# Attention and two expert layers on one core: chunks of 256 instead of 384 tokens, another order of the attention, and K, V and weights brought in differently

## What is computed

```
B, H, S, D = 2, 8, 768, 64; block, window = 32, 16
k_sum = max of k over blocks of 32;  v_sum = mean of v over blocks of 32       # 24 of each
scores = [q k^T / 8 inside |i-j| < 16, else -1e9 ;  q k_sum^T / 8 + log(32)]
x = softmax(scores) @ [v ; v_sum]            -> 1536 tokens x 512
h = relu(x @ w_in)      (512 -> 2048);  y = (h * h) @ w_out        (2048 -> 512)
h2 = y @ w2_in          (512 -> 1024);  solu = h2 * softmax(h2)
out = layernorm(solu) * g @ w2_out           (1024 -> 512)
```

## Time and profile before

| | before |
|---|---|
| median of 3 runs | 531.06 us |
| span of the profiled execution | 529.4 us |
| TensorE busy (share of span) | 492.2 us (93%) |
| VectorE, ScalarE, GpSimd busy | 268.0, 223.8, 36.2 us |
| first layer pair (the chunks' matmuls) begins to run without a gap | about 62.7 us |
| third layer begins | 378.7 us |

### The profile page before, as it was taken

How to read it: one execution, slowest core, us unless ns; L and a number is a source line. 1 busy time by engine, 2 the same in 40 slices (tenths; PEclk the granted TensorE clock), 3 DMA queues, 4 the chain that set the end, 5 groups by cost and what they waited for, 6 DMA issues and landing times.

```text
span 529.4 us, 8722 instructions
## 1 busy us (share of the span) xinstructions
PE 492.2 (93%) x3088; PEld 436.5 (82%) x3088; DVE 268.0 (51%) x548; ACT 223.8 (42%) x553; POOL 36.2 (7%) x45
## 2 busy tenths in 40 slices
PE   3346699999999999999999999999999999999997
PEld 2235499999989999989999999999987888888875
DVE  5456276576575455564644454355374444444330
ACT  3345366556464444453443443333243233333331
POOL 0005411211100000000000000000010000000000
PEclk9966599999999999999999999999999999999999
DMA  7367453342450311232210034222062112211011
GB/s 228 114 207 273 140 156 87 120 140 79 138 181 36 95 36 64 87 133 93 79 40 1 1 104 165 69 61 59 21 195 64 60 62 79 78 60 59 22 39 40
DMA packets 29783, 49.82 MB, mean 94 GB/s; under 512 B 2272, under 2 KB 16864, under 8 KB 29248
## 3 DMA queue, kind: packets, MB, share of 16 engines
q1 hardware_dynamic: 23424, 30.65, 18.9%
q10 hardware_dynamic: 4608, 8.39, 5.4%
q0 software_dynamic: 1728, 10.49, 5.3%
HBM read 40.08 MB, written 9.44 MB: 94 GB/s over the span
## 4 chain that ended last, share of the span: by engine, by line
PE 91%; issue 4%; DVE 2%; DMA 1%; ACT 0%; SPq 0%; ACTq 0%
PE bank L790 27%; PE bank L765 26%; PE bank L896 13%; PE bank L917 13%; PE bank L726 5%; PE bank L746 3%; PE bank L735 2%; PE bank L908 2%; DMA v_raw<-vT 1%; DMA q_sb<-qT 0%; DVE k_ext L535 0%; PE bank L754 0%; DVE k_sum L540 0%; DVE neg_max L557 0%; DVE probs L553 0%
## 5 line engine op out<-in xcount | busy, mean ns | idle before, releaser
L790 PE MATMUL bank<-h_hi,wout_hi 128*128 128x384 f32 x256 | 91.1, 356 | 0.4 <-DVE h_lo L610 0.4
L765 PE MATMUL bank<-x_hi,win_hi 128*128 (+1 forms) x256 | 90.2, 352 | 0.8 <-DVE x_lo L574 0.8
L765 PE MATMUL bank<-x_hi,win_lo 128*128 (+1 forms) x256 | 86.9, 339 | 0.0
L765 PE MATMUL bank<-x_lo,win_hi 128*128 (+1 forms) x256 | 86.8, 339 | 0.0
L790 PE MATMUL bank<-h_hi,wout_lo 128*128 128x384 f32 x256 | 86.4, 337 | 0.0
L790 PE MATMUL bank<-h_lo,wout_hi 128*128 128x384 f32 x256 | 86.1, 336 | 0.0
L409 ACT ACTIVATE relu<-bank 128x384 f32<-128x384 f32 x64 | 31.4, 490 | 103.4 <-PE bank L765 101.4
L607 DVE TENSOR_TENSOR relu<-relu 128x384 f32<-128x384 f32 x64 | 35.7, 558 | 64.9 <-ACT h_hi L414 64.9
L355 ACT ACTIVATE probs<-probs,neg_max 128x118 f32<-128x118 f32 x96 | 36.8, 384 | 42.7 <-DVE neg_max L557 42.7
L790 PEld LDWEIGHTS bank<-h_hi,wout_hi 128*128 128x128 f32 x256 | 48.0, 188 | 5.1 <-issue 3.9
L726 PE MATMUL bank<-k_ext,q_sb 64*64 64x118 f32 x384 | 31.4, 304 | 21.8 <-issue 16.1
(11 more groups left out here) (66 smaller groups left out, 776.7 us busy)
## 6 DMA issues: line engine op xcount, KB each, us to landing
wstage<-wtiles ACTq DMA_DIRECT2D x32, 256.0 KB, 2.7
k_raw<-kT SPq DMA_DIRECT2D x16, 399.0 KB, 3.1
v_raw<-vT SPq DMA_DIRECT2D x16, 384.0 KB, 3.4
v_ext<-vwin SPq DMA_DIRECT2D x16, 282.0 KB
w_in_raw<-w_in_c POOLq DMA_DIRECT2D x4, 1024.0 KB, 6.8
q_sb<-qT SPq DMA_DIRECT2D x16, 192.0 KB, 9.3
y_dram<-x_hi POOLq DMA_DIRECT2D x4, 768.0 KB, 3.8
y_dram<-x_lo POOLq DMA_DIRECT2D x4, 768.0 KB, 4.7
```

The lines of the kernel that those rows point to most:

```text
L765: last = nc.tensor.matmul(bank[:, 6 + f % 2, 0:CH], win[a][:, f * WC + k * P:f * WC + (k + 1) * P], rhs, start=(k == 0 and a == 0 and b == ...
L790: last = nc.tensor.matmul(bank[:, 2 + d, 0:CH], wout[a][:, f * WC + d * P:f * WC + (d + 1) * P], h[b][:, f % 2, :], start=(f == 0 and a == ...
```

## The change

What it does:

- CH is 256 instead of 384, so there are 6 chunks of 16 slices, and every `up` and `down` is 12 matmuls of 256 columns. A unit of attention is one pair of heads and one chunk (TPU = 4 tiles; 24 units).
- Four units come first, then the scores of a fifth. The other attention work stands in `SLOTS`: at slice-steps 0, 4, 7, 10, 13 and from 16 on at each fourth, values of unit a, scores of unit c and transposes of unit b, one behind the other.
- `up(n + 2)` is issued in step n ahead of `down(n)`; `h_hi` and `h_lo` have three slots, the squares of VectorE a buffer `sqr` of their own.
- K is loaded once a batch and pair; windows and summaries of K are spread by GpSimd. V's block sums come from a table `vblk` in which 96 partitions hold the blocks of four pairs; the means are spread into `v_ext` by transfers from `v_mean`; TensorE's turning of the sums and ScalarE's spreading fall away.
- All weights of the first layer pair are loaded whole from SyncE's queue in groups of two tiles (512 KB), into the memory of their own low parts, and the low part is written over the raw one (GpSimd for `w_in`, VectorE for `w_out`, ScalarE the high parts). The third layer's weights come the same way, a group after each two `up` of the last chunk.
- Tiles 8 to 11 of the third layer read y where it was made; only the first four chunks go through DRAM.
- All loops are written out; every engine runs straight code.

The core of the diff (the functions of VectorE and ScalarE for a unit keep their operations, on 4 tiles in place of 3; a line "..." marks what is left out):

```diff
-CH = 384
+CH = 256
-TPJ = CH // QT
-TPU = 3
+TPU = CH // QT
+UNITS = PPB * NCHUNK
+SLOTS = {0: (None, 4, 5), 4: (4, 5, 6), 7: (5, 6, 7), 10: (6, 7, 8), 13: (7, 8, 9)}
+for _u in range(8, UNITS):
+    SLOTS[4 * (_u - 4)] = (_u, _u + 1 if _u + 1 < UNITS else None, _u + 2 if _u + 2 < UNITS else None)
...
 # SyncE's queue
+            load_k(0, 0)
+            load_q(0)
+            sp.dma_start(mask[:, :], mask_c).then_inc(mask_in, 16)
+            load_k(0, 1)
+            sp.dma_start(ident[:, :], ident_c).then_inc(ident_in, 16)
+            load_vf(0)
+            load_q(1)
+            load_vf(1)
+            load_k(0, 2)
+            load_q(2)
+            load_vw(0)
+            load_k(0, 3)
+            load_q(3)
+            load_vw(1)
+            load_w(win_raw, w_in_t, 0, win_in)
+            load_vw(2)
+            load_vw(3)
+            sp.wait_ge(vmean_ok, 1)
+            for p in range(PPB):
+                spread_v(p)
+            sp.wait_ge(scores_ok, 1)
+            load_q(4)
+            load_w(wout_raw, w_out_t, 0, wout_in)
+            load_w(win_raw, w_in_t, 1, win_in)
...
 # ScalarE
+            def hidden(n):
+                act.wait_ge(up_ok, n + 1)
+                if n >= 2:
+                    act.wait_ge(sq_ok, n - 1)
+                nc.scalar.activation(relu[:, n % 2, :], up_bank(n), ACT.Relu).then_inc(relu_ok, 1)
...
+            def x_high(u):
+                c, p = u // PPB, u % PPB
+                act.wait_ge(attn_ps, u + 1)
+                if c >= 2:
+                    act.wait_ge(y_saved[c % 2], 32 * (c // 2))
...
 # TensorE
+            def values(u):
+                c, p = u // PPB, u % PPB
+                pe.wait_ge(vw_in[p], 16 * (c + 1))
+                pe.wait_ge(vs_in[p], 16 * (u // UPB + 1))
+                pe.wait_ge(probsT_ok, u + 1)
+                if u >= 1:
+                    pe.wait_ge(xlo_ok, u)
...
+            scores(0)
+            scores(1)
+            turned(0)
+            scores(2)
+            turned(1)
+            values(0)
+            scores(3)
+            turned(2)
+            values(1)
+            turned(3)
+            values(2)
+            scores(4)
+            up(0, range(0, 2))
+            values(3)
+            up(0, range(2, 3))
+            up(1, range(0, 3))
+            up(0, range(3, 4))
+            up(1, range(3, 4))
+            for n in range(STEPS - 2):
+                if n in SLOTS:
+                    a, b, c = SLOTS[n]
+                    if a is not None:
+                        values(a)
+                    if c is not None:
+                        scores(c)
+                    if b is not None:
+                        turned(b)
+                up(n + 2)
+                down(n)
```

More of the change, by code:

```diff
@@ L159, in build, with scores_bank, up_bank, down_bank @@
         o_ps, o_ok = sem("o_ps"), sem("o_ok")
[L160 to L209, removed]
+        def scores_bank(u):
+            return bank[:, 0 if u % 2 == 0 else 3, 0:UC]
+        probsT_bank = bank[0:KX, 1, 0:TPU * P]
+        xT_bank = bank[:, 2, 0:CH]
+        def up_bank(n):
+            return bank[:, 6 + n % 2, 0:CH]
+        def down_bank(d):
+            return bank[:, 4 + d // 2, (d % 2) * CH:(d % 2 + 1) * CH]
+        def h2_bank(i):
+            return bank[:, 2 * (i % 2):2 * (i % 2) + 2, :].rearrange("p b c -> p (b c)")
+        lnT_bank = bank[:, 6:8, :].rearrange("p b c -> p (b c)")
+        def tile_cols(f):
+            return slice(f * WC, (f + 1) * WC)
         block = ctx.enter_context(nc.Block())
@@ L248, in _ @@
[L248 to L259, removed]
@@ new lines, in store @@
+            def store(i):
+                sp.wait_ge(o_ok, i + 1)
+                sp.dma_start(out[i * P:(i + 1) * P, :], o_sb[:, i % 2, :]).then_inc(o_out[i % 2], 16)
+            sp.wait_ge(xlo_ok, UNITS)
+            for c in range(2):
+                sp.wait_ge(y_saved[c], 32)
+            load_y(0)
+            load_y(1)
+            for g in range(F1 // WG):
+                load_w2(g)
+            for c in range(2):
+                sp.wait_ge(y_saved[c], 64)
+            for i in range(TT):
+                if 2 <= i + 2 < (NCHUNK - 2) * TPC:
+                    sp.wait_ge(h2_ok, i + 1)
+                    load_y(i + 2)
+                store(i)
@@ new lines, in _ @@
+            windows_k(4)
+            w_in_low(0)
+            w_in_low(1)
+            windows_k(5)
+            w_in_low(2)
+            w_in_low(3)
+            for n in range(LAST):
+                if n % F1 == 0 and n:
+                    save_y(n // F1 - 1)
+                if n + 4 < F1:
+                    w_in_low(n + 4)
+                if n in SLOTS and SLOTS[n][2] is not None and SLOTS[n][2] + 1 < UNITS:
+                    u = SLOTS[n][2] + 1
+                    if UPB <= u < UPB + PPB:
+                        summaries_k(1, u - UPB)
+                    windows_k(u)
@@ new lines, in _ @@
+            w_in_high(1)
+            x_high(2)
+            x_high(3)
+            exps(4)
+            w_in_high(2)
+            w_out_high(0)
+            hidden(0)
+            w_in_high(3)
+            w_out_high(1)
+            hidden(1)
+            for n in range(STEPS):
+                if n % F1 == 0 and n:
+                    chunk_y(n // F1 - 1)
+                if n in SLOTS:
+                    a, b, c = SLOTS[n]
+                    if b is not None:
+                        copy_probsT(b)
+                    if a is not None:
+                        x_high(a)
+                if n - 1 in SLOTS and SLOTS[n - 1][2] is not None:
+                    exps(SLOTS[n - 1][2])
+                if n + 2 < STEPS:
+                    hidden(n + 2)
+                if n + 2 < F1:
+                    w_out_high(n + 2)
+                if n + 4 < F1:
+                    w_in_high(n + 4)
+                if n >= LAST + 2:
+                    w2_high(n - LAST - 2)
@@ new lines, in _, with scores @@
+            win, wout, x, h = (win_hi, win_lo), (wout_hi, wout_lo), (x_hi, x_lo), (h_hi, h_lo)
+            def scores(u):
+                c, p = u // PPB, u % PPB
+                pe.wait_ge(q_in[p], 16 * (c + 1))
+                pe.wait_ge(kwin_ok, u + 1)
+                pe.wait_ge(kbc_ok, (u // UPB) * PPB + p + 1)
+                if u >= 2:
+                    pe.wait_ge(masked_ok, u - 1)
+                out_ = scores_bank(u)
+                for t in range(TPU):
+                    for e in range(2):
+                        rows = slice(e * D, (e + 1) * D)
+                        last = nc.tensor.matmul(out_[e * QT:(e + 1) * QT, t * KX:(t + 1) * KX],
+                                                q_sb[rows, p, t * QT:(t + 1) * QT],
+                                                k_ext[rows, p, t * KX:(t + 1) * KX],
@@ new lines, in down @@
+            def down(n):
+                c, f = n // F1, n % F1
+                if c == 0:
+                    pe.wait_ge(wout_lo_ok, f + 1)
+                pe.wait_ge(hlo_ok, n + 1)
+                for d in range(KD):
+                    if f == 0 and c and d % 2 == 0:
+                        pe.wait_ge(yclo_ok, 2 * c - 1 + d // 2)
+                    for a, b in PASSES:
+                        last = nc.tensor.matmul(down_bank(d), wout[a][:, f * WC + d * P:f * WC + (d + 1) * P],
+                                                h[b][:, n % 3, :],
+                                                start=(f == 0 and a == 0 and b == 0 and d % 2 == 0),
+                                                stop=(f == F1 - 1 and a == 1), skip_group_check=True)
+                last.then_inc(down_ok, 1)
```

992 lines of the change are left out of this document (436 added, 556 removed).

## The result

The changed kernel takes 582.11 us (median of 4 runs, 579.98 to 583.03) where the kernel before takes 531.17 (4 runs, 530.66 to 532.26): ratio 1.094, 95% interval 1.092 to 1.096. It is 51 us slower; the forecast was 517, the range 504 to 531. The profiled execution has a span of 578.2 us.

The account below looks back on a forecast made before the run. Until the start ends latencies and transfers decide, then the distance between matmuls. Start 53 + matmuls 268.4 + attention 43.1 + chunk waits 2 + third layer 148.6 = 515.1, plus 1.7 from profiled run to median: 517 us, range 504 to 531.

Parts of the forecast that it names:

- Third layer: The last stage: same matmuls and transposes a tile, nothing waiting for squares or weights, so 148.6 us as before.
- Hand-overs: Chunk starts, where the first x_high waits for y's transfers: just holds, 2 us in all, bounds 0 and 8.
- rival 3: Waits of 3 us a chunk boundary and 3 in the first chunk, or 0.122 a matmul: 524 to 528, chance 0.2.
- signs named as wrong: Pieces of 12 matmuls above 1.49; TensorE idle for ReLU or low parts every sixteenth step; start over before 45 or after 60.
- Start: Before the step loop: transfers decide, values(0) waits until 35.5 us, then 17.5 more, so the loop starts at 53.
- Matmuls: Step loop: 2280 matmuls of 256 columns at 0.1177 us each, 268.4 us; 262 at 0.115, 278 at 0.122.
- The line through two sizes: Price of a 256-column matmul drawn from the measured 384 and 512 columns: 0.1177 us, the value taken.
- the upper bound: Price of a 256-column matmul keeping the 384-column excess of 0.0155 as a fixed cost: 0.122 us.
- The load as the floor: A weight load takes 0.11 us beneath one matmul, so it can be the floor, under 0.1177 by 7%.
- Attention: Beside the step loop's matmuls: 20 units at 2.2 us, less 0.9 for missing scores, 43.1 us; bounds 39 and 54.
- Up two steps ahead: Step loop: two steps, 5.6 us, cover the chain behind an up, so the old 2.4 us gap before the last chunk's first down goes.
- ScalarE in the first chunk: ScalarE needs 2.9 us a step where TensorE needs 3.5, so its work is covered, by 0.6 only.

Follow-up runs that it names:

- x1_yload: The changed kernel with SyncE's third-layer queue storing tile i - 2, not tile i, before it loads y of tile i + 3: 540.56 us.
- b2_store: b1_pad with the changed kernel's third-layer SyncE order (load of tile i + 2, store of tile i, load of tile i + 3): 588.35 us.
- x7_ypad: x1_yload with the V rows of the windows padded from 94 to 96 partitions, attention left at its own steps: 521.5 us.
- x3_both: The changed kernel with the later store of x1_yload and attention at steps 4, 7, 10, 13 of a chunk instead of 0, 4, 8, 12: 529.52 us.
- c1_narrow: x3_both with matmuls of 192 columns in up and 240 in down from the second chunk on, part of the result not computed: 515.53 us.
- c2_apart: x3_both with a slot's attention apart: scores ahead of up, transposes between up and down, values behind down: 546.81 us.
- x6_sums: x5_start with VectorE's sums of K for the second batch one step earlier: 512.4 us.
- b1_pad: The kernel before the change with the V rows of the windows padded from 94 to 96 partitions, nothing else: 512.69 us.
- x5_start: x4_pad with the start reordered so that scores and transposes of later units run ahead of the first values: 514.65 us.
- x4_pad: x3_both with the V rows of the windows padded on the host from 94 to 96 partitions: 520.92 us.

## Why the prediction was wrong, and where it held

**Third layer: the step that failed.** "Same 48 matmuls and 8 transposes a tile ... 148.6 again." It walked TensorE's work, the weights' split and VectorE's maximum, and not SyncE's queue, though the diff rewrites the loop that fills it. Two lines of code and the earlier trace rows would have been enough: a tile takes some 12 us (two products of 5.60 and the transposes), `store(i)` can go out only when tile i is done, `load_y(i + 3)` is behind it, issue and landing are some 5 us, and tile i + 3 is due at once, because TensorE runs ahead. None of the rivals had it. `x1_yload` takes the loss away, `b2_store` makes it: shown from both sides. It is 38.8 of the 63 us missed.

**Hand-overs: mechanism right, size wrong.** The order ScalarE, ReLU, TensorE, its place (each sixteenth step) and the thin margin stood in the text; rival 3 gave it 3 us a boundary. ScalarE was to be free 7 us after the last `down` and was so after 11.3. Landing was taken as 4 us, from the 4.7 of the earlier trace rows for more bytes; it was 8.1 to 9.0. The text had the two slow engines for the start and did not ask what else is on them when y goes out: a `vwin` load issued in the same step. `x7_ypad` shows it, and so does `x3_both`, where no `vwin` load is issued beside y and its low part lands in 3.7, 4.1 and 5.1 us at the same three hand-overs: about the 4 us that had been reckoned. And a TensorE that stands still for 4 us gets the clock back late, a cost that the sum held only for the start: 6.2 of the 16.9 us. The point is one of the signs named as wrong, idle time put down to ReLU at every sixteenth step, here at three of the four.

**Start: right to 0.6 us, with a wait behind it that the sum did not have.** `values(0)` was put at 35.5 and ran at 36.78, with the DMA engines at a tenth and 33 to 66 GB/s from 22 to 27 us; padding moved it by 8. The rest was to take 17.5 and took 16.8. But `turned(4)`, in the loop's first slot, then waited for VectorE's normalisation, which stood behind the low part of the first `w_out` (1.34), and at 58.6 the clock fell for 3.3 us. The prediction's walk of the first chunk looked at ScalarE alone; its rival 3 had 3 us there.

```profile
53.56 1.03 PE L699 MATMUL bank<-k_ext,q_sb 64*64 64x118 f32 x16
57.38 0.66 PE L712 MATMUL bank<-ident,probs 128*118 128x128 f32 x4 [2.79 <-DVE probs L547]
```

**Matmuls: right within its bounds.** 12 in 1.44 us and not 1.41, 0.120 where the text had 0.115, 0.1177 and 0.122. The line through two sizes undershot by 0.0023; the upper bound, a fixed cost on top of the columns, was 0.002 too high. 5.2 us over 2280. The load as the floor at 0.110 was right, and 0.010 below. The Trainium skill, TensorE: Matmul & The Clock Gate, Part 3, The mechanism, says in one line that loads overlap matmuls only where the row groups differ, and in another that a load into the background weight buffer is pulled ahead too. `c1_narrow` contradicts the first again, with 0.110 a pair where load plus stream would be 0.19; the second would fit.

**Attention: right.** 2.15 a full unit against 2.2, and `c2_apart` gives the 0.24 that a unit saves by standing in one place. The chain of the changed kernel, one unit:

```profile
71.03 0.62 PE bank L725 x16
71.64 0.96 PE bank L699 x16
72.60 0.58 PE bank L712 x4
```

**Up two steps ahead, ScalarE in the first chunk: right.** No `down` waits for ReLU or squares, and behind its first slot the first chunk's steps have no gap.

**What the change is worth without its faults.** Its own structure costs 2304 x 0.120 = 276.5 us of matmul where 1536 x 0.1755 = 269.6 stood, and gives back attention and the gap of 2.4. `x6_sums`, all faults removed, is 512.4; `b1_pad`, the kernel before with two partitions of zeros, is 512.7. Both are some 3.5% under the kernel before, and no difference between them is shown. The largest gain of all runs was in one transfer's shape, open to the old kernel as well. That the two run equally fast through different stages is measured; that a start like that of `x5_start` in the kernel before would put it ahead is not tried.

## What to carry to other kernels

Walk every queue in program order, not only the engine that bounds the kernel: a load issued behind a store that waits for compute is as late as that compute. Before anything else, look in the DMA view for stretches at a tenth or two of the engines, and make the partition count of such a transfer a multiple of 16; ask also which other transfers share its engines. Price a stillstand of TensorE with the slow matmuls that follow it.

## What the runs showed of the hardware

- A load on two engines delays others that use all sixteen: y's landing went from 9.04 to 5.52 us when a `vwin` load of 188 KB beside it was padded by 4 KB. The issuing queue is held up too: behind the first two `vwin` loads of the start one issue of SyncE took 5.43 us and the next two 5.75 (below); in `x4_pad` the same took 0.43 and 3.00.

```profile
11.10 5.43 SPq L208 DMA_DIRECT2D win_raw<-w_in_t  x1
16.57 5.75 SPq L194 DMA_DIRECT2D v_ext<-vwin  x2
```

- After stillstands of 2.8 to 5.8 us TensorE ran at half the clock for about 3 to 6 us: 8.4 us of loss for a wait of 5.4 in `b2_store`. Behind the waits of 1.1 to 1.4 us in `x3_both` the granted clock stayed at 1.00 (147 to 150 and 160 to 163 us).
- A matmul of type fp32r with its own weight load, start to start: 0.110 us at 192 columns, 0.1135 at 240, 0.120 at 256, 0.1755 at 384, 0.2333 at 512. The load is hidden down to about 230 columns (0.110 less 0.0135 at 2.4 GHz, worked out from these).
- A change between matmuls of the big and of the attention's form costs about 0.2 us there and back, 0.24 a unit in `c2_apart`.
